# Fused attention and two MoE blocks on one Trainium2 core: in the second block w_out2's features take other partitions, ScalarE centres all tiles, one low part is moved

## Reference

```python
# x: output of attention (8 x 8 heads x 576 x 64, by way of 32 packed rows) and of a first MoE block
def _moe2_ref(x, w_in, w_out, g_ln):          # x 4608x512, w_in 512x1024, w_out 1024x512, g_ln 1024
    h = x @ w_in
    h_max = np.max(h, axis=-1, keepdims=True)
    e = np.exp(h - h_max)
    sm = e / (np.sum(e, axis=-1, keepdims=True) + 1e-09)
    solu = h * sm
    mu = np.mean(solu, axis=-1, keepdims=True)
    var = np.mean((solu - mu) ** 2, axis=-1, keepdims=True)
    ln = (solu - mu) / np.sqrt(var + 1e-06) * g_ln
    return (ln @ w_out).astype(np.float32)
```

## Time and profile before

| what | value |
|---|---|
| median of 3 runs | 1180.65 us (1177.53 to 1190.14) |
| profiled execution | 1181.89 us |
| its span (first to last instruction) | 1180.1 us |
| TensorE (PE) busy | 1124.4 us, 95% |
| VectorE (DVE) busy | 1055.8 us, 89% |
| ScalarE (ACT) busy | 871.1 us, 74% |
| GpSimd (POOL) busy | 416.6 us, 35% |

### The profile page before, as it was taken

The page is one execution under the profiler, slowest core; times in us unless marked ns, Lnnn a source line. Parts: engine busy times, 40 slices in busy tenths (PEclk is TensorE's granted clock), DMA queues, the critical chain, the costliest instruction groups (busy, mean ns, idle before and its releaser), DMA issues.

```text
span 1180.1 us, 22774 instructions
## 1 busy us (share of the span) xinstructions
PE 1124.4 (95%) x8480; PEld 998.3 (85%) x8480; DVE 1055.8 (89%) x1686; ACT 871.1 (74%) x1366; POOL 416.6 (35%) x284
## 2 busy tenths in 40 slices
PE   5878889999999999999999999999999999999998
PEld 3444558999999999999999999997688888888876
DVE  6998989999999999999999999988878787887872
ACT  4576798888888888888888888754657566665752
POOL 2443324343342333433334334244434243343200
PEclk9898999999999999999999999999999999999999
DMA  9998963221212122111122021121453535445441
GB/s 336 393 381 310 330 258 116 75 62 33 85 49 75 29 66 85 39 56 57 49 74 66 30 84 39 57 80 48 151 171 124 187 116 178 142 157 163 127 151 44
DMA packets 92896, 149.69 MB, mean 127 GB/s; under 512 B 9856, under 2 KB 56960, under 8 KB 92800
## 3 DMA queue, kind: packets, MB, share of 16 engines
q1 hardware_dynamic: 92800, 148.41, 37.7%
HBM read 91.23 MB, written 57.15 MB: 126 GB/s over the span
## 4 chain that ended last, share of the span: by engine, by line
PE 57%; DVE 21%; DMA 10%; issue 6%; ACT 4%; POOL 0%; DVEq 0%; ACTq 0%; SPq 0%; POOLq 0%
PE ps_y L73 11%; PE ps_y L75 11%; PE ps_y L74 11%; PE ps_h L73 6%; PE ps_h L75 6%; PE ps_h L74 6%; DMA c_raw<-c_scratch 5%; DVE terms L1816 5%; DVE solu L1805 4%; DMA c_scratch<-terms 4%; DVE stats L1793 2%; ACT c_hi L1635 1%; DVE kT L639 1%; ACT terms L1607 1%; PE ps_o L73 1%
## 5 line engine op out<-in xcount | busy, mean ns | idle before, releaser
L1072 POOL TENSOR_TENSOR den<-den,h_abs 128x576 f32<-128x576 f32 x128 | 223.7, 1748 | 389.2 <-ACT den L1025 389.1
L73 PE MATMUL ps_y<-g_hi,wout_hi 128*128 128x288 f32 x1024 | 303.2, 296 | 1.7 <-ACT wp_out L572 1.7
L74 PE MATMUL ps_y<-g_lo,wout_hi 128*128 128x288 f32 x1024 | 302.1, 295 | 0.0
L75 PE MATMUL ps_y<-g_hi,wout_lo 128*128 128x288 f32 x1024 | 301.1, 294 | 0.0
L73 PEld LDWEIGHTS ps_y<-g_hi,wout_hi 128*128 128x128 f32 x1024 | 191.9, 187 | 1.9 <-ACT wp_out L572 1.9
L75 PEld LDWEIGHTS ps_y<-g_hi,wout_lo 128*128 128x128 f32 x1024 | 192.9, 188 | 0.0
L74 PEld LDWEIGHTS ps_y<-g_lo,wout_hi 128*128 128x128 f32 x1024 | 192.3, 188 | 0.0
L73 PE MATMUL ps_h<-x_hi,wp_hi 128*128 128x288 f32 x512 | 152.2, 297 | 1.2 <-DVE wp_lo L1087 1.1
L74 PE MATMUL ps_h<-x_lo,wp_hi 128*128 128x288 f32 x512 | 151.1, 295 | 0.0
L75 PE MATMUL ps_h<-x_hi,wp_lo 128*128 128x288 f32 x512 | 150.5, 294 | 0.0
L1019 ACT ACTIVATE h_abs<-ps_h 128x576 f32<-128x576 f32 x128 | 83.3, 651 | 83.3 <-PE ps_h L75 83.2
(11 more groups left out here) (172 smaller groups left out, 2505.6 us busy)
## 6 DMA issues: line engine op xcount, KB each, us to landing
wp_scratch<-wp_out SPq DMA_DIRECT2D x32, 512.0 KB, 6.0
wp_lo<-wp_scratch SPq DMA_DIRECT2D x32, 512.0 KB, 4.2
c_scratch<-terms SPq DMA_DIRECT2D x32, 512.0 KB, 2.8
c_raw<-c_scratch SPq DMA_DIRECT2D x32, 512.0 KB, 4.3
k_main<-in_k SPq DMA_DIRECT2D x16, 576.0 KB, 7.2
q_main<-in_q SPq DMA_DIRECT2D x16, 576.0 KB, 6.9
v_main<-in_v SPq DMA_DIRECT2D x16, 576.0 KB, 7.4
y_scratch<-y_out SPq DMA_DIRECT2D x16, 576.0 KB, 3.4
```

What stands on the lines that cost most here:

```text
L73: pe.matmul(out, lh, rh, start=first, stop=False)
L74: pe.matmul(out, lh, rl, start=False, stop=False)
L75: return pe.matmul(out, ll, rh, start=False, stop=last)
L1072: pool.tensor_tensor(den[s % 3][:, :, :], den[s % 3][:, :, :], h_abs[:, :, :], ALU.mult)\
```

## The change

- *Placement.* Partition 4x + a now holds the eight features 256a + 32f + x, f from 0 to 7, instead of 8p to 8p + 7. Then the 32x32 blocks that VectorE turns are of 32 neighbouring columns: `by_blocks` is gone, `turn_blocks` reads `solu` as it lies. The DMAs to and from c_scratch stay as they are.
- *Loads.* Each of the four slices of w_out2 comes by four DMAs of 128 KB (one for each a, to every fourth partition). The gain comes by four DMAs of single elements. `coef_in` is waited for at 96 instead of 48, `slice_in` at four times as much for w_out2.
- *Plain couples.* ScalarE centres them too, from `solu` to `terms`, and there puts the columns in the order that the transposes want: it writes every fourth column. The transposes and the square read `terms`. VectorE's second instruction in `weighted` is gone. The exponential of couple 1 now waits for the transposes of couple 0, and `weighted` of couple 1 for its centring.
- *Last step.* On ScalarE `centre` of 34 comes ahead of `high` of 32, then the exponential of 35, the square of 34, `high` of 33, `emit` of 31 and `centre` of 35. On VectorE the low part of tile 31 is no longer at the end of the step before, but behind `inverse` in the last step.

```diff
@@ -1008,7 +1008,7 @@
             split_block_hi(act, 0, n, k)
 
     def magnitudes(act):
-        act.wait_ge(coef_in, 48)
+        act.wait_ge(coef_in, 96)
         act.activation(b_abs[:, :], ab[:, 4:6], ACT.Abs).then_inc(coef, 1)
         act.wait_ge(coef, 3)
 
@@ -1092,7 +1092,7 @@
             split_block_lo(dve, 0, n, k)
 
     def coefficients_in(dve):
-        dve.wait_ge(coef_in, 48)
+        dve.wait_ge(coef_in, 96)
 
     def numerator(dve, s):
         n, h = num[s % 4][:, :, :], ps_h[s % 2]
@@ -1176,9 +1176,12 @@
     y_d = y_scratch.rearrange("kt p n -> p kt n")
     win_d = w_in2.rearrange("(kt p) f -> p kt f", p=P)
-    wout_d = w_out2.rearrange("(p ft) n -> p ft n", p=P)
+    QUARTER = PACK // FT2
+    wout_d = w_out2.rearrange("(a f x) n -> a x f n", f=FT2, x=PACK)
+    gain_d = gain.rearrange("(a f x) -> a x f", f=FT2, x=PACK)
     RING = 4
     COUPLES = TILES // 2
     LAST = COUPLES - 1
@@ -1304,10 +1307,6 @@
     def is_couple(c, j, u):
         return isinstance(c, int) and 2 * c + j == u
 
-    def by_blocks(i):
-
-        return solu[i].rearrange("p (x n) -> p n x", n=PACK)
-
     def c_arrived(i):
 
         return c_raw[i].rearrange("p (t f x) -> p f t x", t=P // PACK, f=FT2)
@@ -1337,13 +1336,16 @@
         return [w[n - KT][:, half] for w in (win_hi, win_lo)]
 
     def gain_to_sbuf(sp):
-        sp.dma_start(gain_in[:, :], gain.rearrange("(p ft) -> p ft", p=P)).then_inc(rational["coef_in"], 16)
+        for a in range(QUARTER):
+            sp.dma_start(gain_in[a::QUARTER, :], gain_d[a], allow_slow_non_contiguous=True)\
+                .then_inc(rational["coef_in"], 16)
 
     def slice_load(sp, n):
 
         if n < KT:
-            sp.dma_start(stage.rearrange("p (a n) -> p a n", a=2), wout_d[:, 2 * n:2 * n + 2, :])\
-                .then_inc(slice_in, 16)
+            for a in range(QUARTER):
+                sp.dma_start(stage[a::QUARTER, :].rearrange("p (f n) -> p f n", f=2), wout_d[a][:, 2 * n:2 * n + 2, :])\
+                    .then_inc(slice_in, 16)
         else:
             sp.dma_start(stage, win_d[:, n - KT, :]).then_inc(slice_in, 16)
 
@@ -1373,7 +1375,7 @@
             hi, _ = slice_parts(n, h)
             raw = stage[:, h * DM:(h + 1) * DM]
             if h == 0:
-                act.wait_ge(slice_in, 16 * (n + 1))
+                act.wait_ge(slice_in, 16 * QUARTER * (n + 1) if n < KT else 16 * (QUARTER * KT + n - KT + 1))
             if n < KT:
                 act.activation(hi, raw, ACT.Copy, scale=gain_in[:, 2 * n + h:2 * n + h + 1]).then_inc(slice_hi_ready, 1)
             else:
@@ -1501,9 +1503,8 @@
             pe.wait_ge(centred, k + 1)
             if i == 1:
                 pe.wait_ge(c_lo_ready, k)
-            columns = solu[i].rearrange("p (q f) -> p f q", f=FT2)
             for ft in range(FT2):
-                mm = pe.transpose(ps_t[:, ft, :], columns[:, ft, :], ident[:, :])
+                mm = pe.transpose(ps_t[:, ft, :], terms[i][:, ft * P:(ft + 1) * P], ident[:, :])
             mm.then_inc(turned, 1)
 
         def output(pe, c, j, i, back, part):
@@ -1604,18 +1605,25 @@
             act.wait_ge(nmax_ready, k + 1)
             wait_for(act, solu_ready, k - 1)
             wait_for(act, c_stored[i], 16 * (2 * c + j - back - 1))
+            if is_couple(c, j, 1 + back):
+                act.wait_ge(turned, i + 1)
             act.activation(terms[i], h, ACT.Exp, bias=nmax[t], accum_out=total[t]).then_inc(terms_ready, 1)
 
         def centre(act, c, j, i, back):
             k, t = RING * c + 2 * j + i - 2 * back, 2 * ((j + back) % 2) + i
             act.wait_ge(nmean_ready, k + 1)
-            act.activation(solu[i], solu[i], ACT.Identity, bias=nmean[t]).then_inc(centred, 1)
+            if on_tensor(c, j, back):
+                act.activation(terms[i].rearrange("p (f x a) -> p a f x", f=FT2, x=PACK),
+                               solu[i].rearrange("p (a f x) -> p a f x", f=FT2, x=PACK),
+                               ACT.Identity, bias=nmean[t]).then_inc(centred, 1)
+            else:
+                act.activation(solu[i], solu[i], ACT.Identity, bias=nmean[t]).then_inc(centred, 1)
 
         def square(act, c, j, i, back):
             k, t = RING * c + 2 * j + i - 2 * back, 2 * ((j + back) % 2) + i
             act.wait_ge(centred, k + 1)
             wait_for(act, squared, k)
-            act.activation(squares, solu[i], ACT.Square, accum_out=square_sum[t]).then_inc(squared, 1)
+            act.activation(squares, terms[i] if on_tensor(c, j, back) else solu[i], ACT.Square, accum_out=square_sum[t]).then_inc(squared, 1)
 
         def root(act, c, j, back):
             u, s = 2 * c + j - back, (j + back) % 2
@@ -1679,6 +1687,7 @@
                 rational["y_to_sbuf_act"](act, CHUNKS - 1, 1)
                 exponentials(act, c, j, 0, 0)
                 sums_high(act, 0, 1)
+                centre(act, c, j, 0, 0)
                 square(act, c, j, 0, 0)
                 w_high(act, 3)
                 high(act, c, j, 0, 0)
@@ -1686,6 +1695,7 @@
                 return
             if is_couple(c, j, 1):
                 first_product_out(act, c, j)
+                centre(act, c, j, 1, 1)
                 square(act, c, j, 1, 1)
                 root(act, c, j, 1)
                 for i in range(2):
@@ -1704,11 +1714,13 @@
                 emit(act, c, j, 0, 2)
                 exponentials(act, c, j, 0, 0)
                 root(act, c, j, 1)
+                centre(act, c, j, 0, 0)
+                high(act, c, j, 0, 1)
+                exponentials(act, c, j, 1, 0)
                 square(act, c, j, 0, 0)
-                exponentials(act, c, j, 1, 0)
-                high(act, c, j, 0, 1)
+                high(act, c, j, 1, 1)
                 emit(act, c, j, 1, 2)
-                high(act, c, j, 1, 1)
+                centre(act, c, j, 1, 0)
                 return
             first_product_out(act, c, j)
             centre(act, c, j, 0, 1)
@@ -1798,7 +1810,7 @@
             w = solu[i]
             dve.wait_ge(terms_ready, k + 1)
             if is_couple(c, j, 1 + back):
-                dve.wait_ge(turned, i + 1)
+                dve.wait_ge(centred, i + 1)
             elif not is_couple(c, j, back):
                 dve.wait_ge(blocks_turned, k - 3)
             wait_for(dve, squared, k - 1)
@@ -1806,14 +1818,11 @@
                                      accum_out=solu_sum[t]).then_inc(solu_ready, 1)
             dve.wait_ge(solu_ready, k + 1)
             dve.tensor_scalar(nmean[t], solu_sum[t], -1.0 / FF2, None, ALU.mult).then_inc(nmean_ready, 1)
-            if direct:
-                dve.wait_ge(nmean_ready, k + 1)
-                dve.tensor_scalar(w, w, nmean[t], None, ALU.add).then_inc(centred, 1)
 
         def turn_blocks(dve, c, j, i, back):
             k = RING * c + 2 * j + i - 2 * back
             dve.wait_ge(centred, k + 1)
-            dve.transpose(terms[i].rearrange("p (n x) -> p n x", n=PACK), by_blocks(i)).then_inc(blocks_turned, 1)
+            dve.transpose(terms[i], solu[i]).then_inc(blocks_turned, 1)
 
         def inverse(dve, c, j, back):
             u, s = 2 * c + j - back, (j + back) % 2
@@ -1924,6 +1933,7 @@
             weighted(dve, c, j, 1, 1)
             inverse(dve, c, j, 1)
             if is_couple(c, j, LAST):
+                low(dve, c, j, 1, 2)
                 turn_blocks(dve, c, j, 0, 1)
                 turn_blocks(dve, c, j, 1, 1)
                 largest(dve, c, j, 0, 0)
@@ -1944,7 +1954,8 @@
             scaling(dve, c, j, 1)
             c12(dve, c, j)
             low(dve, c, j, 0, 1)
-            low(dve, c, j, 1, 1)
+            if not is_couple(c, j, LAST - 1):
+                low(dve, c, j, 1, 1)
 
         couples(step)(dve)
         c, j = COUPLES // 2 - 1, 1
```

## The result

The changed kernel takes **1172.95 us** (median of 20 runs, 1169.15 to 1183.83), the kernel before, run beside it, 1180.41 (20 runs). The ratio is 0.9931 [0.9912, 0.995]: 0.7% faster, 7.5 us between the medians. The profiled execution has a span of 1171.3 us against 1180.1, 8.8 us less.

A forecast was written before the change was run, and what follows sets the result against it. The loop was taken as bound by TensorE. Terms 1.2 + 0.9 + 0.6 + 2.5 + 3.6 = 8.8 us off the 1180.1 us span gave 1171.3, a median of 1171.8 us; range 1165.0 to 1178.5.

The forecast's parts named there:

- The loop, 2.5: Third stage, thirteen loop steps: faster turns remove the delays and TensorE's waits for u3, gaining 2.5 us.
- 0.6 at 852.84: Third stage, before the loop: TensorE's wait for u3 at 852.84 goes with the faster turns, 0.6 us.
- The step of couple 2, 0.9: Stage's start: the second turn's own 0.93 us shortens TensorE's waits of 832.50 and 839.10, together 0.9 us.
- The centring, 1.2: Stage's start: centring on ScalarE starts TensorE's transposes 1.05 us sooner, plus about 0.2 at product 7; 1.2 us.
- The last step, 3.6: Last step: TensorE's gap before the output of tile 32 goes, 2.0 us, and the clock's fall with it, 1.6.
- now three things work: Last step: shorter turns (1.86), an earlier start (1.86 and about 1.2) and ScalarE's new order close the 2.0 us gap.
- The clock, 1.6 at 7 in 10: Last step: the fall to 1.2 GHz behind TensorE's gap goes with it, 1.6 us, given seven chances in ten.
- rival A: Clock falls at the end all the same, or stepped centring costs 2.0 us: 1173.4 (both 1174.1); chance 0.22.
- The transfers, 0: Split loads of w_out2 and gain: extra issues and single elements fit the available room; cost 0, at most 3.2 us.
- Rival D: Gain load: single elements stall the key and weight loads, making the kernel slower, 1184.9 at 230 ns each; chance 0.05.
- B: Turns stay at 2.12 us, being bound elsewhere: only 4.8 us gained, 1175.9; chance 0.08.
- C: Stage's start: waits of 848.07 and 805.35 go too, some 4 us more gained, 1168; chance 0.12.

The follow-up runs named there:

- turn_alone: The kernel before with only its 32 turns on neighbouring columns; 1174.69 us, ratio to before 0.9941.
- better: The changed kernel with two ScalarE orders altered: first step's square behind high parts and exponential, couple 2's second centring ahead of the sum's high part; 1171.37 us.
- old_tail: The changed kernel with the last step's old order on both ScalarE and VectorE; 1175.74 us, ratio 0.9951.
- slow_turn: The changed kernel with its 32 turns stepping over 32 columns again; 1179.4 us, ratio to before 0.9949.
- gap3: The changed kernel plus a TensorE wait for the low part of tile 34 before the output of tile 32; 1180.19 us.
- slow_old_tail: The changed kernel with stepped turns and the last step's old order, leaving the move of the centring; 1182.52 us.
- centre_vector: The changed kernel with plain tiles centred on VectorE instead of ScalarE, with the same stepped write; 1173.18 us.
- gap2: The changed kernel plus a TensorE wait for an evicted result (tile 31's emit) before the output of tile 32; 1177.32 us.
- gain_one: The changed kernel with the gain loaded by one DMA as before; 1173.94 us, ratio 0.9941.
- tail_alone: The kernel before with only the last step's new order, low part of tile 31 moved too; 1177.51 us.

## Why the prediction was right, and where its terms were not

The forecast was 8.8 us off the span and 1171.8 us; measured were 8.8 and 1172.95, within 1% as given the chance of 0.80. The total is better than its parts deserve: part I gave 1.56 where 2.1 were forecast (1.2 and 0.9), part II 3.61 where 3.1 were (2.5 and 0.6), part III 3.82 where 3.6 were.

- **The loop, 2.5, and 0.6 at 852.84.** Mechanism right: the wait for u3 is gone, TensorE loses nothing in II, and turn_alone has the whole of it. The size was 3.6 for the two together. I took 0.227 us a matmul from ten rows; the loop after, 265.22 us over 13 x 90 matmuls, gives 0.2267. Over 1,170 matmuls the rounding is 0.4 us, nearly all that was missing. The other three kernels with slow turns have a II of 269.22 to 269.53, so the price of the slow turns itself varies by 0.7.
- **The step of couple 2, 0.9.** Part I falls by 1.1 with the turns alone, and the wait of 832.50 is gone. Right, within the scatter of part I.
- **The centring, 1.2.** The term that failed is "I take 1.5" and its bounds, 1.15 to 2.0: 2.13 us measured. I had the price by two routes, one through the turn's ratio (2.0) and one through an activation of 64 columns, and chose a value between them near the second. Its 285 ns for 64 columns say little of the columns: 1,144 ns for 1,024 make 0.9 ns a column and leave some 0.23 us for the rest of the instruction (an estimate from the two rows). The Trainium skill's note on 16-byte lines (SBUF — State Buffer, "Door 1: The DMA port swizzle") pointed to the upper end, and the runs agree with it: 2.13 written with a step and 2.17 read with one, against 1.14 without. The second thing that failed there is who ends the wait of 805.35. I had the high part's chain on ScalarE end it at 804.3. In the changed kernel ScalarE's high part ends at 803.70, and VectorE's queue (two w_diff_lo, the maximum) at 803.79, so the low part ends at 804.95 by either; better, with ScalarE's part sooner, keeps the wait. What I did not ask is what comes on VectorE in the place of the centring: w_diff_lo, slowed there by 1.9 us (rows under better), so VectorE gained 0.6 us and not 2.45. What the move gives in part I is about 0.5 where 1.2 was forecast (53.64 against turn_alone's 54.11, less than the scatter; the two pairs with stepped turns give 0.07 and 0.96), and in the old order it costs 0.7 to 1.1 in part III.
- **The last step, 3.6.** Measured 3.82, and "now three things work" is wrong as a reason. Turns alone give 3.74, the order alone (the moved low part with it) 3.74, and the moved low part nothing where the rest is in place. I had summed reliefs (1.86, 1.86, 1.2) against a gap of 2.0 and did not ask which single one would have been enough. I had also named the maximum of tile 35 as what ends last; in the changed kernel it ends at 1139.34 and the low part waits until 1140.19, for ScalarE's high part behind the long centring. For a centring of 2.0 the prediction had 2.1 us to spare, and 1.95 were measured. That the two are not both needed is also why taking one away (old_tail, slow_turn) shows so little: the effect of a part depends on what else is in place. What the new order really does in the changed kernel is to make the long centring harmless: without it, 1.0 us of gap.
- **The clock, 1.6 at 7 in 10.** It followed a gap in gap3, slow_old_tail and centre_vector, at a price of 1.6 us; a gap of 1.7 us did not bring it (gap2). Of rival A's two conditions one came true, the long centring, and the other, the fall all the same, did not. What part I lacked, 0.5, was made up by the loop's 0.5 and the last step's 0.2, so the right total rests in part on errors that cancel.
- **The transfers, 0.** Right in the sum. The issues cost 4.5 us and not 1.9, and the room of 3.1 us would not have held them. It did not matter, because the key load landed no later than before, although it was issued 4 us later. The DMA engines were busy without a break from 11 to 19 us in both kernels, so transfers ahead of it may decide its landing; no run separates that from the later issue of the loads behind it. The sixteen loads of w_out2 have no run of their own; the third stages of after and before began 0.2 us apart, within the scatter. Rival D fell. The rule of the Trainium skill (DMA: Bandwidth & Descriptors, "Rules for kernel authors"), one descriptor per element, is borne out by the count: gain_one has 944 packets fewer than after, near the 1,024 elements, but they had no price that shows here.
- **Rivals B and C.** Turns are 1.23 us, so B fell; its side remark, that the order alone would bring the low part in time, holds (tail_alone, 2.3 us to spare). C asked for the waits of 805.35 and 848.07 to go; they show 0.37 us (0.53 before) and 0.63 (0.50 before).

What stays open: why turns of the same length cost 3.6 us of part II in one execution and 4.0 to 4.3 in three others; what slows VectorE's instruction at the stage's start; and whether the four gain loads cost a few tenths at the start.

## What to carry to other kernels

Where two edits each close the same gap, test each alone from the kernel before and each removed from the kernel after: here both directions were needed, and one of them alone would have credited the wrong edit. Cut the trace at instructions that all kernels share; the length of part II told differences of 0.1 us where the whole time told only differences of several. A move to an idle engine pays nothing if the operation gets slower there by the step of its access; look at the order behind it before crediting the move.

## What the runs showed of the hardware that was not expected

- An activation of 1,024 columns costs 1.0 us more (2.13 and 2.17 against 1.14) with a step on either side; VectorE's centring with the same stepped write takes 1.13 to 1.17 us against 0.75 in place (the first of the four, beside GpSimd, 2.85 against 2.45); the turn 2.12 against 1.23.
- SP's issue of a DMA of 256 single elements takes 1.13 us (4.53 for four), an issue of rows 0.43.
- A key load issued 4 to 5 us later landed no later, at 23.55 against 24.1 and 24.3.
- In the third stage, while TensorE had work, the granted clock fell from 2.4 to 1.2 GHz only behind the four longer idle times listed under gap3, each time 0.4 to 0.7 us after work had resumed, for 3.4 us, and 1.6 us were lost by it.
- At the stage's start, beside GpSimd's y_sum_lo, VectorE's instruction takes 1.7 to 1.9 us more: the centring 2.45 us against 0.75, w_diff_lo 3.13 against 1.2. In the loop the two turns beside the same operation of GpSimd are not slowed (2.36 us for both at 865.94).
